# A gated scan and two feed-forward layers on one core: the first tile's blocks in a new order

## The chip, the cores and the metric

The kernel runs on 1 core of one Trainium2 chip. The metric is the device time of one execution in microseconds (us). Before the change the median of 3 runs is 1988.1 us (1988.08 to 1988.46).

## What is computed

```python
# x, f_logit: (2, 6080, 256) float32; lower_bound: (256,)
f = lower_bound + (1 - lower_bound) * sigmoid(f_logit)
h = 0
for t in range(6080):                 # one state per sequence and channel
    h = f[:, t] * h + (1 - f[:, t]) * x[:, t]
    y[:, t] = h
y = y.reshape(12160, 256)
h1 = y @ w_in1                        # 256 x 2048
y1 = (h1 - tanh(h1)) @ w_out1         # 2048 x 256
h2 = y1 @ w_in2
out = max(0.01 * h2, h2) @ w_out2
```

All of it is float32. Each float32 product is made of three matmuls: an operand is split into a rounded part (`_hi`) and the rest (`_lo`), and hi*hi, hi*lo and lo*hi are summed in PSUM.

## The kernel before, in words

Channels lie on the partitions (256 channels are two halves, k = 0 and 1), tokens on the free axis. A tile holds the same stretch of tokens of both sequences, b = 0 (A) and b = 1 (B): 448 of each in the first tile, 512 in the 11 others. Layer 1 runs over tiles 0 to 11 and writes `y1` to HBM, layer 2 over tiles 12 to 22 and the last. The 2048 hidden channels are 8 groups of 2 x 128, f = 0 and 1. A group of a tile so has four blocks (f, b) of 128 hidden channels by one sequence's tokens: C11 = (0, 0), C22 = (1, 1), C21 = (1, 0), C12 = (0, 1), numbered 0 to 3 in this order (lines 29 and 30).

From tile 1 on, the four blocks of a group come from seven products of sums of weights and of inputs (`slot`, line 362). The first tile does without them: `plain_block` (line 427) makes a block of two half-blocks, one for each k, of three matmuls each, so eight products for a group. Its four blocks have four PSUM banks: `p_ps`, `q_ps` and the two of `x_ps`. Then, for each block:
- ScalarE takes tanh of the bank into `full` (`plain_bend`, L594);
- VectorE subtracts it from the bank (`make_plain_g`, L914), after which the bank is free for the next group;
- ScalarE rounds `full` to `g_hi` (`round_g`, L619);
- VectorE writes the rest to `g_lo` (`split_g`, L878);
- TensorE multiplies with `w_out` and adds to the four banks of `y_ps` (`outputs`, L346 to L348): two outputs of three matmuls for each block.

Weights come from HBM as float32 and are split too: `plain_w_round` (L522, L523) and `plain_w_split` (L884, L886) for the plain part of `w_in`, `wo_round` (L538) and `wo_split` (L906) for `w_out`. GpSimd makes the sums of `w_in` that later tiles want (`sum_weights`, L1048 to L1053), rounded and split by `sum_w_round` (L527) and `sum_w_split` (L892). SyncE issues the loads, in a written order (lines 241 to 272): `load_wi(n)` waits, from n = 3 on, for `sum_w_split(n - 3)`, because there are three staging buffers; `load_wo(n)`, from n = 2 on, for `wo_split(n - 2)`.

Every engine runs a list in a fixed order, written by hand as slots, one for each group. In the first tile (`plain_slot`, lines 449, 634 and 918) TensorE does for group g: C11, then the outputs of C11 of group g - 1, then C22 and its outputs, C21, C12. Slot 0 has no outputs; TensorE begins with `WARM` matmuls on zeros and puts `FILL` more between the blocks of sequence A and those of B (L447).

Ahead of it stands the scan of the first tile, unit by unit (a unit is a k and a b; `FIRST_ORDER` takes both units of sequence A first): load of logits and x (`first_unit`, line 201), tanh (`first_squash`, L492), the gate's scale and shift (`first_forget_gate`, L501), (gate - 1) * x (`drive_term`, L768), the scan (L782), rounding and split of the result (L549, L828). The units of the next tile are interleaved with slots 1 to 4: `squash` (L509), `forget_gate` (L515), `drive_term` and `scan`, and behind them in slots 5 and 6 `keep_states` and the sums of inputs (L796, L803, L810) that tile 1 wants; `x_round` (L572) and `x_split` (L822) follow in slot 7.

The 8 weights W21 of the first tile are kept in the places of `x_hi` and `x_lo` that T3 and T1 take in tile 1 (`w21_place`), so their rounding must wait for the last blocks that read them.

```python
            def plain_slot(g):                     # TensorE, L449
...
                else:
                    for c in (C11, C22, C21, C12):
                        plain_block(g, c)
                        outputs(0, g - 1, c, 0, W_FIRST)
                        outputs(0, g - 1, c, 1, W_FIRST)
```

Of the kernel before, what the change touches and what calls it, by code (L numbers as in the profile page):

```python
# [8 lines left out]
WARM = 34  # L9
GROUPS = 8  # L10
# [24 lines left out]

FIRST_ORDER = (0, 2, 1, 3)
X12 = T4
FIRST_DONE = {C11: 1, C21: 2, C22: 3, C12: 4}
FILL = 12


def gated_scan_ffn_kernel(
# [41 lines left out]
    def plain_count(g, c):  # L84
        return FIRST_DONE[c] if g == 0 else 4 * g + c + 1

# [8 lines left out]
    with ExitStack() as ctx:  # L95
# [36 lines left out]
        bound_in = sem("bound_in")  # L132
        consts_ready = sem("consts_ready")
# [43 lines left out]

        block = ctx.enter_context(nc.Block())

        @block.sync  # L180
        def _(sp):
# [61 lines left out]
            load_wi(0)  # L243
            first_unit(2)
            first_unit(3)
            load_wi(1)
# [10 lines left out]
            load_wo(4)  # L257
            load_wi(5)
            load_unit(1, 3)
            load_wo(5)  # L260
            load_wi(6)
            load_unit(2, 0)
            load_wo(6)
            load_wi(7)
            load_unit(2, 1)
            load_wo(7)
# [66 lines left out]
        def _(pe):  # L333
# [16 lines left out]
            def outputs(s, g, c, k, W):  # L350
                q = 8 * s + g
                if k == 0:
                    pe.wait_ge(g_split, 4 * q + c + 1)
# [8 lines left out]
            def slot(s, g):  # L362
# [19 lines left out]
                if second and g == 0:  # L382
                    pe.wait_ge(full_ready, 4 * (GROUPS - 1) + C21 + 1)
                elif second and g == 1:
                    pe.wait_ge(full_ready, 4 * (GROUPS - 1) + C12 + 1)
# [23 lines left out]
                if not (second and g == 0):  # L409
                    pe.wait_ge(c12_ready, n)  # L410
# [13 lines left out]
            def plain_bank(c):  # L424
                return {C11: p_ps[:, :W_FIRST], C22: q_ps[:, :W_FIRST], C21: x_ps[:, 0, :W_FIRST], C12: x_ps[:, 1, :W_FIRST]}[c]

            def plain_block(g, c):
                f, b = BLOCK_OF[c]
                bank = plain_bank(c)
                if g >= 1:  # L430
                    pe.wait_ge(full_ready, 4 * (g - 1) + c + 1)
                if f == 0:
                    weights = [(wi_hi[:, g, W11, :], wi_lo[:, g, W11, :]), (wi_hi[:, g, W12, :], wi_lo[:, g, W12, :])]
                else:
                    weights = [(w21_place(x_hi, g), w21_place(x_lo, g)), (wi_hi[:, g, W22, :], wi_lo[:, g, W22, :])]
                inputs = (X11, X21) if b == 0 else (X12, X22)
                for k in range(2):
                    hi, lo = weights[k]
                    i = inputs[k]
                    nc.tensor.matmul(bank, hi, x_hi[:, i, :W_FIRST], start=k == 0, stop=False)  # L440
                    nc.tensor.matmul(bank, hi, x_lo[:, i, :W_FIRST], start=False, stop=False)
                    mm = nc.tensor.matmul(bank, lo, x_hi[:, i, :W_FIRST], start=False, stop=k == 1)
                mm.then_inc(plain_done, 1)
# [4 lines left out]

            def plain_slot(g):  # L449
                pe.wait_ge(plain_w_ready, g + 1)  # L450
                if g == 0:
                    pe.wait_ge(x_ready, 2)
                    plain_block(g, C11)
                    plain_block(g, C21)
                    warm(FILL)
                    pe.wait_ge(x_ready, 4)
                    plain_block(g, C22)
                    plain_block(g, C12)
                else:
                    for c in (C11, C22, C21, C12):  # L460
                        plain_block(g, c)
                        outputs(0, g - 1, c, 0, W_FIRST)
                        outputs(0, g - 1, c, 1, W_FIRST)
# [7 lines left out]

            for g in range(GROUPS):
# [15 lines left out]
        def _(act):  # L488
# [7 lines left out]
            def first_forget_gate(i):  # L496
                j = FIRST_ORDER[i]
                if i == 0:
# [52 lines left out]
            def x_round(s, i):  # L551
                W = width(s)
                act.wait_ge(sums_ready, sums_count(s) + 3)
                if isinstance(s, int) and s == 1:
                    act.wait_ge(plain_done, plain_count(GROUPS - 1, C12 if i in (T4, X22) else C21))
# [33 lines left out]
            def plain_bend(g, c):  # L589
                bank = {C11: p_ps[:, :W_FIRST], C22: q_ps[:, :W_FIRST], C21: x_ps[:, 0, :W_FIRST], C12: x_ps[:, 1, :W_FIRST]}[c]  # L590
                act.wait_ge(plain_done, max(plain_count(g, c), plain_count(g, C22)) if g == 0 and c == C21 else plain_count(g, c))
                if g >= 1:
                    wait_split(g - 1, c)
                nc.scalar.activation(full[:, c, :W_FIRST], bank, ACT.Tanh).then_inc(bent_ready, 1)  # L594
# [6 lines left out]
            def wait_split(n, c):  # L601
                act.wait_ge(g_split, 4 * n + c + 1)

            def begun(s, g, back):
                return not (isinstance(s, int) and 8 * s + g < back)

            def bend(s, g, c, W):
                q = 8 * s + g
                wait_block(q, c)
                if begun(s, g, 1):  # L610
                    wait_split(q - 1, c)
                nc.scalar.activation(full[:, c, :W], block_source(g % 2, c, W), ACT.Tanh).then_inc(bent_ready, 1)  # L612

            def round_g(s, g, c, W):
                q = 8 * s + g
                act.wait_ge(full_ready, 4 * q + c + 1)
                if begun(s, g, 2):
                    act.wait_ge(g_used, 4 * (q - 2) + c + 1)
# [15 lines left out]
            def plain_slot(g):  # L634
                if g >= 1:
# [471 lines left out]
```

## Time and profile before

| | |
|---|---|
| median of 3 runs | 1988.1 us |
| the profiled execution | 1988.08 us, its span 1986.3 us |
| TensorE (PE) busy | 1969.9 us, 99% of the span |
| weight loads of TensorE (PEld) | 1632.2 us, 82% |
| VectorE (DVE) | 1586.6 us, 80% |
| ScalarE (ACT) | 1247.8 us, 63% |
| GpSimd (POOL) | 39.6 us, 2% |
| HBM | 36 GB/s over the span |

The span runs from the first to the last instruction of the program; the time of the execution holds 1.8 us more. All places in time below are counted from the start of the span. PE is the matmul part of TensorE. Matmuls are pipelined: their recorded ends overlap the starts of the next ones, so their pace is read from start to start.

### The profile page before, as it was taken

How to read it: one execution, taken by the hardware profiler on the slowest of the kernel's cores; microseconds unless marked ns; L12 is line 12 of the kernel's file. 1: busy time of each engine (PE TensorE's matmuls, PEld its weight loads, DVE VectorE, ACT ScalarE, POOL GpSimd, SP SyncE). 2: the span in 40 equal slices, each digit the busy share in tenths (PEclk: the TensorE clock that was granted, in tenths of full speed). 3: DMA queues.
4: the chain of work that ended last, by engine and by line, in shares of the span. 5: the costliest groups of instructions: out<-in, count | busy, mean ns of one | idle time of the engine just before them, and what ended most of it. 6: DMA issues, size and time to landing. Idle time of an engine off the chain costs nothing.

```text
span 1986.3 us, 28715 instructions
## 1 busy us (share of the span) xinstructions
PE 1969.9 (99%) x8710; PEld 1632.2 (82%) x8710; DVE 1586.6 (80%) x2481; ACT 1247.8 (63%) x2205; POOL 39.6 (2%) x69
## 2 busy tenths in 40 slices
PE   8999999999999999999999999999999999999999
PEld 6888888888888888888888888888888888888887
DVE  6788888888888888888788777787777877878776
ACT  5577777777777777777665455554555545545454
POOL 1200000000000000000110000000000000000000
PEclk9999999999999999999999999999999999999999
DMA  3210110101101011011021010110101101011000
GB/s 122 64 51 22 54 43 21 53 32 42 42 21 63 23 41 42 21 69 40 21 75 40 6 43 1 42 42 0 42 0 42 42 0 42 0 42 42 0 21 21
DMA packets 38216, 71.14 MB, mean 36 GB/s; under 512 B 3360, under 2 KB 5920, under 8 KB 38176
## 3 DMA queue, kind: packets, MB, share of 16 engines
q1 hardware_dynamic: 38176, 70.66, 10.5%
q8 instruction: 18, 0.29, 0.1%
q14 instruction: 22, 0.18, 0.0%
HBM read 45.75 MB, written 24.90 MB: 36 GB/s over the span
## 4 chain that ended last, share of the span: by engine, by line
PE 96%; DVE 2%; ACT 1%; issue 0%; DMA 0%; SPq 0%; ACTq 0%; DVEq 0%
PE y_ps L346 17%; PE y_ps L347 17%; PE y_ps L348 17%; PE x_ps L336 8%; PE x_ps L337 8%; PE x_ps L338 8%; PE q_ps L336 4%; PE q_ps L337 4%; PE q_ps L338 4%; PE p_ps L336 2%; PE p_ps L337 2%; PE p_ps L338 2%; DVE g_lo L878 1%; DVE full L914 0%; DVE raw L782 0%
## 5 line engine op out<-in xcount | busy, mean ns | idle before, releaser
L619 ACT CAST g_hi<-full 128x512 fp32r<-128x512 f32 (+1 forms) x768 | 473.0, 616 | 265.3 <-DVE full L872 106.6
L878 DVE TENSOR_TENSOR g_lo<-full,g_hi 128x512 fp32r<-128x512 f32 (+1 forms) x768 | 508.1, 682 | 139.0 <-ACT g_hi L619 134.8
L346 PE MATMUL y_ps<-g_hi,wo_hi 128*128 128x512 f32 (+1 forms) x1536 | 597.2, 389 | 8.8 <-DVE wo_lo L906 8.8
L348 PE MATMUL y_ps<-g_hi,wo_lo 128*128 128x512 f32 (+1 forms) x1536 | 595.8, 388 | 0.0
L347 PE MATMUL y_ps<-g_lo,wo_hi 128*128 128x512 f32 (+1 forms) x1536 | 595.7, 388 | 0.0
L576 ACT COPY part<-x_ps 128x512 f32<-128x512 f32 (+1 forms) x552 | 319.5, 579 | 237.8 <-PE x_ps L338 232.8
L346 PEld LDWEIGHTS y_ps<-g_hi,wo_hi 128*128 128x128 f32 x1536 | 288.9, 188 | 70.5 <-issue 10.6
L348 PEld LDWEIGHTS y_ps<-g_hi,wo_lo 128*128 128x128 f32 x1536 | 289.0, 188 | 57.2
L347 PEld LDWEIGHTS y_ps<-g_lo,wo_hi 128*128 128x128 f32 x1536 | 289.1, 188 | 56.8
L336 PE MATMUL x_ps<-x_hi,wi_hi 128*128 128x512 f32 (+1 forms) x736 | 286.6, 389 | 0.0
L337 PE MATMUL x_ps<-x_lo,wi_hi 128*128 128x512 f32 (+1 forms) x736 | 285.7, 388 | 0.0
L338 PE MATMUL x_ps<-x_hi,wi_lo 128*128 128x512 f32 (+1 forms) x736 | 285.7, 388 | 0.0
L612 ACT ACTIVATE full<-part 128x512 f32<-128x512 f32 x264 | 167.3, 634 | 79.8 <-DVE part L835 68.5
L872 DVE SCALAR_TENSOR_TENSOR full<-part 128x512 f32<-128x512 f32 (+1 forms) x288 | 196.3, 682 | 1.7
L842 DVE TENSOR_TENSOR part<-q_ps,part 128x512 f32<-128x512 f32 (+1 forms) x184 | 126.3, 686 | 88.5 <-PE q_ps L338 85.3
L861 DVE TENSOR_TENSOR full<-part,full 128x512 f32<-128x512 f32 x264 | 181.4, 687 | 8.2 <-ACT full L612 5.1
L336 PEld LDWEIGHTS x_ps<-x_hi,wi_hi 128*128 128x128 f32 x736 | 138.1, 188 | 31.0 <-ACT part L576 2.7
L338 PEld LDWEIGHTS x_ps<-x_hi,wi_lo 128*128 128x128 f32 x736 | 138.1, 188 | 28.1
L337 PEld LDWEIGHTS x_ps<-x_lo,wi_hi 128*128 128x128 f32 x736 | 138.2, 188 | 26.9
L835 DVE TENSOR_TENSOR part<-p_ps,part 128x512 f32<-128x512 f32 (+1 forms) x184 | 126.2, 686 | 35.8 <-PE p_ps L338 35.7
L336 PE MATMUL q_ps<-x_hi,wi_hi 128*128 128x512 f32 (+1 forms) x368 | 143.1, 389 | 0.8 <-DVE part L842 0.7
L338 PE MATMUL q_ps<-x_hi,wi_lo 128*128 128x512 f32 (+1 forms) x368 | 142.8, 388 | 0.0
(95 smaller groups left out, 1790.8 us busy)
## 6 DMA issues: line engine op xcount, KB each, us to landing
gate<-f_logit SPq DMA_DIRECT2D x44, 256.0 KB, 2.7
drive<-x SPq DMA_DIRECT2D x44, 256.0 KB, 2.9
y<-y_out SPq DMA_DIRECT2D x22, 512.0 KB, 2.8
raw<-y SPq DMA_DIRECT2D x22, 512.0 KB, 4.4
out<-y_out SPq DMA_DIRECT2D x21, 512.0 KB, 2.8
wi_stage<-w_in SPq DMA_DIRECT2D x16, 256.0 KB, 3.3
wo_stage<-w_out SPq DMA_DIRECT2D x16, 256.0 KB, 2.8
y_out<-f_logit SPq DMA_DIRECT2D x4, 224.0 KB, 4.6
```

The lines of the kernel that those rows point to most:

```text
L336: nc.tensor.matmul(bank, hi, x_hi[:, i, :W], start=start, stop=False, skip_group_check=True)
L337: nc.tensor.matmul(bank, hi, x_lo[:, i, :W], start=False, stop=False, skip_group_check=True)
L338: return nc.tensor.matmul(bank, lo, x_hi[:, i, :W], start=False, stop=stop, skip_group_check=True)
L346: nc.tensor.matmul(bank, hi, g_hi[:, g % 2, c, :W], start=start, stop=False, skip_group_check=True)
L347: nc.tensor.matmul(bank, hi, g_lo[:, g % 2, c, :W], start=False, stop=False, skip_group_check=True)
L348: return nc.tensor.matmul(bank, lo, g_hi[:, g % 2, c, :W], start=False, stop=stop, skip_group_check=True)
L576: nc.scalar.copy(part[:, par, i, :W], x_ps[:, par, :W]).then_inc(chain_copied, 1)
L612: nc.scalar.activation(full[:, c, :W], block_source(g % 2, c, W), ACT.Tanh).then_inc(bent_ready, 1)
L619: nc.scalar.copy(g_hi[:, g % 2, c, :W], full[:, c, :W]).then_inc(g_hi_ready, 1)
L861: ins = nc.vector.tensor_tensor(full[:, c, :W], h, full[:, c, :W], ALU.subtract)
L872: ins = nc.vector.scalar_tensor_tensor(out=full[:, c, :W], in0=h, scalar=LEAK, in1=h, op0=ALU.mult, op1=ALU.max)
L878: nc.vector.tensor_tensor(g_lo[:, par, c, :W], full[:, c, :W], g_hi[:, par, c, :W].bitcast(F32), ALU.subtract).then_inc(g_split, 1)
```

## The change

The blocks of the first tile are put in a new order, and every engine's list with them:
- In the slots 1 to 6 TensorE makes C11 and C21 (sequence A) of group g + 1 and C22 and C12 (sequence B) of group g; each is followed by the outputs of C11 and C21 of group g, and of C22 and C12 of group g - 1. `FIRST_BLOCKS` and `FIRST_OUTPUTS` list both orders; `made` and `used` turn a block into the count at which it is done.
- The start is cut into half-blocks: those that read X11 alone come first, then those with X21, then C11 and C21 of group 1, then the blocks of B. So that C11 and C21 of groups 0 and 1 can be there at once, group 1 has two banks of `y_ps` and two places of `part` for them.
- `WARM` goes from 34 to 24 and the 12 `FILL` matmuls go.
- The gate of unit 0 is made by VectorE (`first_gate`), and the load of `bound` is issued by ScalarE instead of SyncE.
- SyncE's order: `load_wi(1)` ahead of units 2 and 3, each `load_wo(n + 1)` ahead of `load_wi(n + 1)`, one place earlier than before.
- On ScalarE and VectorE `wo_round` and `wo_split` come for group g + 1 in slot g, the weights of `w_in` for group g + 2, the drive of the next tile at the end of slots 1 to 4, its scans in slots 2 to 5.
- GpSimd's sums of group g wait for block C22 of group g - 1 (for g = 0: C21 of group 1) instead of C22 of group g.
- `x_round` of tile 1 waits for the new counts.

The diff, cut to its core:

```diff
-WARM = 34
+WARM = 24
-FIRST_DONE = {C11: 1, C21: 2, C22: 3, C12: 4}
-FILL = 12
+FIRST_BLOCKS = [(0, C11), (0, C21), (1, C11), (1, C21), (0, C22), (0, C12)]
+FIRST_OUTPUTS = [(0, C11), (0, C21)]
+for _g in range(1, GROUPS - 1):
+    FIRST_BLOCKS += [(_g + 1, C11), (_g, C22), (_g + 1, C21), (_g, C12)]
+    FIRST_OUTPUTS += [(_g, C11), (_g - 1, C22), (_g, C21), (_g - 1, C12)]
...
+    def made(q, c):
+        return FIRST_BLOCKS.index((q, c)) + 1 if isinstance(q, int) and q < GROUPS else 4 * q + c + 1
...
+        def plain_bank(g, c):
+            if g == 1 and c in (C11, C21):
+                return y_ps[:, (C11, C21).index(c), 1, :W_FIRST]
...
# SyncE
-                if i == 0:
-                    sp.dma_start(bound[:, :], lower_bound).then_inc(bound_in, 16)
             first_unit(0)
             first_unit(1)
             load_wi(0)
+            load_wi(1)
             first_unit(2)
             first_unit(3)
-            load_wi(1)
...
             load_wo(2)
+            load_wo(3)
             load_wi(3)
-            load_wo(3)
+            load_wo(4)
             load_wi(4)
...
# TensorE
+            def first_slots():
+                pe.wait_ge(plain_w_ready, 1)
+                pe.wait_ge(x_ready, 1)
+                plain_half(0, C11, 0)
+                plain_half(0, C21, 0)
+                pe.wait_ge(x_ready, 2)
+                plain_half(0, C11, 1)
+                plain_half(0, C21, 1)
+                pe.wait_ge(plain_w_ready, 2)
+                plain_block(1, C11)
+                plain_block(1, C21)
+                pe.wait_ge(x_ready, 3)
+                plain_half(0, C22, 0)
+                plain_half(0, C12, 0)
+                pe.wait_ge(x_ready, 4)
+                plain_half(0, C22, 1)
+                plain_half(0, C12, 1)
+                plain_outputs(0, C11)
+                plain_outputs(0, C21)
             def plain_slot(g):
+                if g + 1 < GROUPS:
+                    pe.wait_ge(plain_w_ready, g + 2)
+                    plain_block(g + 1, C11)
+                    plain_outputs(g, C11)
+                plain_block(g, C22)
+                plain_outputs(g - 1, C22)
+                if g + 1 < GROUPS:
+                    plain_block(g + 1, C21)
+                    plain_outputs(g, C21)
+                plain_block(g, C12)
+                plain_outputs(g - 1, C12)
# ScalarE
             def plain_slot(g):
+                if g + 1 < GROUPS:
+                    plain_bend(g + 1, C11)
+                plain_round_g(g - 1, C12)
+                sum_w_round(g - 1)
...
+                plain_bend(g, C22)
+                if g + 1 < GROUPS:
+                    plain_round_g(g + 1, C11)
+                    wo_round(g + 1)
+                    plain_bend(g + 1, C21)
...
+                plain_round_g(g, C22)
+                if g + 2 < GROUPS:
+                    plain_w_round(g + 2)
...
+                plain_bend(g, C12)
+                if g + 1 < GROUPS:
+                    plain_round_g(g + 1, C21)
...
                 if g in (1, 2, 3, 4):
                     squash(1, g - 1)
                     forget_gate(1, g - 1)
...
+            act.dma_start(bound[:, :], lower_bound).then_inc(bound_in, 16)
             first_squash(0)
-            first_forget_gate(0)
             first_squash(1)
             first_forget_gate(1)
             plain_w_round(0)
             first_x_round(X11, 0, 0)
+            plain_w_round(1)
+            first_x_round(X21, 2, 1)
             first_squash(2)
...
# VectorE
+            def first_gate():
...
+                nc.vector.tensor_scalar(
+                    y_out[:, b, k, :W_FIRST], y_out[:, b, k, :W_FIRST], gate_scale[:, k:k + 1], gate_shift[:, k:k + 1],
+                    ALU.mult, ALU.add,
+                ).then_inc(first_gate_ready, 1)
             def plain_slot(g):
+                if g + 1 < GROUPS:
+                    make_plain_g(g + 1, C11)
+                split_plain_g(g - 1, C12)
+                sum_w_split(g - 1)
+                if g in (2, 3, 4, 5):
+                    scan(1, g - 2)
...
+                make_plain_g(g, C22)
+                if g + 1 < GROUPS:
+                    split_plain_g(g + 1, C11)
+                    wo_split(g + 1)
+                    make_plain_g(g + 1, C21)
...
+                split_plain_g(g, C22)
...
+                if g + 2 < GROUPS:
+                    plain_w_split(g + 2)
...
+                make_plain_g(g, C12)
+                if g + 1 < GROUPS:
+                    split_plain_g(g + 1, C21)
+                if g in (1, 2, 3, 4):
+                    drive_term(1, g - 1)
...
+            first_gate()
             drive_term(0, 0)
             scan(0, 0)
...
             first_x_split(X11, 0, 0)
             plain_w_split(0)
             first_x_split(X21, 2, 1)
+            plain_w_split(1)
             drive_term(0, 2)
...
+            make_plain_g(0, C11)
             first_x_split(X22, 3, 3)
+            make_plain_g(0, C21)
+            wo_split(0)
+            split_plain_g(0, C11)
+            split_plain_g(0, C21)
...
# GpSimd
-                    pool.wait_ge(plain_done, plain_count(g, C22))
+                    pool.wait_ge(plain_done, made(1, C21) if g == 0 else made(g - 1, C22))
```

## Rows read from the trace of the kernel before

**Rows 1.** The page: a costly group of TensorE, and the issues of w_in

```profile
L346 PE MATMUL y_ps<-g_hi,wo_hi 128*128 128x512 f32 (+1 forms) x1536 | 597.2, 389 | 8.8 <-DVE wo_lo L906 8.8
...
wi_stage<-w_in SPq DMA_DIRECT2D x16, 256.0 KB, 3.3
```

**Rows 2.** Waits of 0 to 110 us: who for whom, sum, times, longest

```profile
DVE drive L768 <- ACT gate L515: 14.3, 4, 3.6
...
PE y_ps L346 <- DVE wo_lo L906: 8.8, 5, 2.0
...
PE p_ps L440 <- DVE wi_lo L886: 1.1, 2, 0.6
```

**Rows 3.** Busy time by stretch

```profile
core 0: us, PE busy (x) PEld busy (x) DVE busy (x) ACT busy (x) POOL busy (x), PEclk, DMA share, GB/s
6.70:11.00 4.30, 4.30 (x21) 1.96 (x20) 4.10 (x8) 3.81 (x8) 0.00 (x0) 1.00 0.98 367
34.00:37.30 3.30, 3.16 (x9) 2.84 (x10) 1.60 (x3) 2.10 (x6) 0.00 (x0) 0.50 0.23 79
60.74:73.49 12.75, 10.23 (x48) 8.85 (x49) 8.10 (x15) 7.02 (x15) 1.76 (x4) 1.00 0.27 84
83.76:93.68 9.92, 9.92 (x50) 9.01 (x48) 8.21 (x15) 5.33 (x12) 2.46 (x4) 1.00 0.09 28
103.60:1986.00 1882.40, 1877.51 (x8305) 1556.09 (x8304) 1515.23 (x2361) 1187.86 (x2087) 21.34 (x32) 1.00 0.10 33
```

**Rows 4.** Timeline of TensorE: start, duration, line, what; idle before and its releaser

```profile
1.32 10.13 PE L447 MATMUL y_ps<-zeros 128*128 128x512 bf16 x34 [1.32 <-POOL zeros L1068]
...
11.10 0.55 PE L440 MATMUL p_ps<-x_hi,wi_hi 128*128 128x448 f32 x1
...
13.72 2.76 PE L447 MATMUL y_ps<-zeros 128*128 128x512 bf16 x12
...
16.13 0.55 PE L440 MATMUL q_ps<-x_hi 128*128 128x448 f32 x1
...
21.38 0.44 PE L346 MATMUL y_ps<-g_hi,wo_hi 128*128 128x448 f32 x1 [1.26 <-DVE wo_lo L906]
...
34.14 0.71 PE L346 MATMUL y_ps<-g_hi,wo_hi 128*128 128x448 f32 x1 [1.98 <-DVE wo_lo L906]
...
60.74 0.44 PE L346 MATMUL y_ps<-g_hi,wo_hi 128*128 128x448 f32 x1 [1.78 <-DVE wo_lo L906]
...
73.49 0.44 PE L346 MATMUL y_ps<-g_hi,wo_hi 128*128 128x448 f32 x1 [1.97 <-DVE wo_lo L906]
...
103.60 0.39 PE L336 MATMUL x_ps<-x_hi,wi_hi 128*128 128x512 f32 x1
```

**Rows 5.** The same timeline: ends of two stretches without a wait

```profile
83.76 0.37 PE L440 MATMUL p_ps<-x_hi,wi_hi 128*128 128x448 f32 x1
...
85.83 0.37 PE L347 MATMUL y_ps<-g_lo,wo_hi 128*128 128x448 f32 x1
...
104.28 0.36 PE L346 MATMUL y_ps<-g_hi,wo_hi 128*128 128x448 f32 x1
...
106.10 0.39 PE L336 MATMUL x_ps<-x_hi,wi_hi 128*128 128x512 f32 x1
```

**Rows 6.** Timelines of VectorE and ScalarE in the start, one later row

```profile
5.48 0.62 DVE L768 SCALAR_TENSOR_TENSOR full<-y_out,full 128x448 f32<-128x448 f32 x1 [1.78 <-DMA full<-x]
6.14 1.09 DVE L782 TENSOR_TENSOR_SCAN raw<-y_out,full 128x448 f32<-128x448 f32 x1
...
9.07 0.62 DVE L828 TENSOR_TENSOR x_lo<-raw,x_hi 128x448 fp32r<-128x448 f32 x1
...
9.81 0.55 DVE L886 TENSOR_TENSOR wi_lo<-wi_stage,wi_hi 128x384 fp32r<-128x384 f32 x1
...
78.83 0.81 DVE L886 TENSOR_TENSOR wi_lo<-wi_stage,wi_hi 128x384 fp32r<-128x384 f32 x1
...
6.00 0.58 ACT L492 ACTIVATE y_out<-y_out 128x448 f32<-128x448 f32 x1 [1.27 <-DMA y_out<-f_logit]
...
7.86 0.30 ACT L522 CAST x_hi<-wi_stage 128x128 fp32r<-128x128 f32 x1 [0.49 <-DMA wi_stage<-w_in]
```

More of the change, by code:

```diff
@@ L176, in gated_scan_ffn_kernel, with plain_full @@
         last_stored = sem("last_stored")
+        def plain_bank(g, c):
+            if g == 1 and c in (C11, C21):
+                return y_ps[:, (C11, C21).index(c), 1, :W_FIRST]
+            return {C11: p_ps[:, :W_FIRST], C22: q_ps[:, :W_FIRST], C21: x_ps[:, 0, :W_FIRST], C12: x_ps[:, 1, :W_FIRST]}[c]
+        def plain_full(g, c):
+            if g == 1 and c in (C11, C21):
+                return part[:, 0, (C11, C21).index(c), :W_FIRST]
+            return full[:, c, :W_FIRST]
         block = ctx.enter_context(nc.Block())
@@ L408, in slot @@
                     pe.wait_ge(x_ready, x_count(s) + 5)
-                if not (second and g == 0):
+                if second and g == 0:
+                    pe.wait_ge(full_ready, made(GROUPS - 1, C22))
+                else:
                     pe.wait_ge(c12_ready, n)
@@ L445, in warm, with plain_outputs @@
+            def plain_block(g, c):
+                ago = made_ago(g, c)
+                if ago is not None:
+                    pe.wait_ge(full_ready, made(*ago))
+                plain_half(g, c, 0)
+                plain_half(g, c, 1)
+            def plain_outputs(g, c):
+                for k in range(2):
+                    if g == 0 and c == C22:
+                        pe.wait_ge(full_ready, made(1, (C11, C21)[k]))
+                    outputs(0, g, c, k, W_FIRST)
             def warm(count):
@@ L470, in _ @@
             warm(WARM)
-            for g in range(GROUPS):
+            first_slots()
+            for g in range(1, GROUPS):
                 plain_slot(g)
@@ L589, in plain_bend, with plain_round_g @@
             def plain_bend(g, c):
[L590 to L594, printed above, removed]
+                act.wait_ge(plain_done, made(g, c))
+                ago = made_ago(g, c)
+                if ago is not None:
+                    act.wait_ge(g_split, made(*ago))
+                nc.scalar.activation(plain_full(g, c), plain_bank(g, c), ACT.Tanh).then_inc(bent_ready, 1)
+            def plain_round_g(g, c):
+                act.wait_ge(full_ready, made(g, c))
+                if g >= 2:
+                    act.wait_ge(g_used, used(g - 2, c))
+                nc.scalar.copy(g_hi[:, g % 2, c, :W_FIRST], plain_full(g, c)).then_inc(g_hi_ready, 1)
             def block_source(par, c, W):
@@ L601, in wait_split @@
             def wait_split(n, c):
-                act.wait_ge(g_split, 4 * n + c + 1)
-            def begun(s, g, back):
-                return not (isinstance(s, int) and 8 * s + g < back)
+                act.wait_ge(g_split, made(n, c))
             def bend(s, g, c, W):
@@ L731, in _ @@
             first_forget_gate(3)
+            plain_bend(0, C11)
             first_x_round(X12, 1, 2)
+            plain_bend(0, C21)
+            wo_round(0)
+            plain_bend(1, C11)
             first_x_round(X22, 3, 3)
-            for g in range(GROUPS):
+            plain_round_g(0, C11)
+            plain_w_round(2)
+            plain_round_g(0, C21)
+            plain_bend(1, C21)
+            wo_round(1)
+            plain_bend(0, C22)
+            plain_round_g(1, C11)
+            plain_bend(0, C12)
+            plain_round_g(1, C21)
+            plain_round_g(0, C22)
+            for g in range(1, GROUPS):
                 plain_slot(g)
@@ L1022, in _ @@
             scan(0, 3)
+            make_plain_g(0, C11)
             first_x_split(X22, 3, 3)
+            make_plain_g(0, C21)
+            wo_split(0)
+            split_plain_g(0, C11)
+            split_plain_g(0, C21)
+            plain_w_split(2)
+            make_plain_g(1, C11)
+            make_plain_g(1, C21)
+            wo_split(1)
+            split_plain_g(1, C11)
+            make_plain_g(0, C22)
+            split_plain_g(1, C21)
+            make_plain_g(0, C12)
+            split_plain_g(0, C22)
             keep_states(0)
-            for g in range(GROUPS):
+            for g in range(1, GROUPS):
                 plain_slot(g)
```

181 lines of the change are left out of this document (80 added, 101 removed).

## The prediction

> **What bounds the kernel now.** I read the page first: the costliest group of TensorE was idle for 8.8 us in the whole run, ended by `wo_split` [rows 1]. The waits of the first 110 us hold the same 8.8 us in 5 waits and 1.1 us in 2 waits for `plain_w_split` [rows 2]. So everything to be had lies in the first tile. Behind it, some 8305 matmuls take 1882.4 us, 0.2267 each, TensorE busy for 1877.5 of them [rows 3], and the change leaves their order alone. Any gain is made before tile 1 and carried unchanged to the end.
>
> The first tile runs from 11.10 to 103.60, where the first three-part product of tile 1 starts [rows 4]: 92.5 us. It has 64 half-blocks and 56 outputs of three matmuls each, 360 in all (24 more outputs run inside tile 1, before and after the change). Their pace, start to start, is 2.07 us for ten in one stretch and 1.82 for nine, 0.202, in another [rows 5]; I take 0.2045 each, so 73.6 us of work. 18.9 us are lost. Where:
> - 12 filling matmuls on zeros, 13.72 to 16.13: 2.4 us [rows 4].
> - Five waits of the outputs: idle 8.8 us; a stall also costs the 0.16 us by which a matmul's end lies behind its successor's normal start (0.36 less 0.20 [rows 5]), so 9.6. Two waits for weights: 1.1 + 2 x 0.16 = 1.4 [rows 2, 4].
> - Three stretches with a granted clock of 0.50, the 1.2 GHz level instead of 2.4. One stands in [rows 3]: 9 matmuls in 3.3 us, 0.37 each, so 9 x 0.168 = 1.5 us lost; the other two look alike, 4.6 together. Each follows one of the long waits, which end at 34.14, 47.43 and 73.49 [rows 4].
> - The rest, 0.9, is slow first matmuls behind stalls.
>
> Why TensorE waits is seen in the slot from 60.74 to 73.49: 12.75 us long, yet VectorE is busy only 8.10 and ScalarE 7.02. The slot from 83.76 to 93.68 has VectorE at 8.21, ScalarE at 5.33, and 9.92 us for the same 48 matmuls without a stall [rows 3]. Neither engine is full; the order makes them wait on each other. In slots 1 to 4 VectorE's `drive_term` stands in line for ScalarE's gate (14.3 us in 4 waits [rows 2]), and behind it everything up to `wo_split`, for which the outputs wait.
>
> **The start, part by part.** The bound's load leaves SyncE's queue, so the x load of unit 0, issued at 1.67, goes 0.48 earlier; first_gate moves that gate from ScalarE to VectorE. VectorE waited for x, not for the gate, until 5.48 [rows 6], so moving the gate is worth nothing: both engines idle there. The earlier issue is worth between 0 and 0.45 us. I take 0.2. The two loads run side by side on the same transfers as before. The Trainium skill ("DMA: Bandwidth & Descriptors", section "Issuing engines are not separate DMA queues") says that starting DMAs from several engines saves only the sequencer's time to initiate. By that rule the worth would be this 0.48 us of issue at most; no row of before shows a second issuer.
>
> From there I walk the two queues, each instruction behind its queue and its wait, with the durations of [rows 6] (drive and splits 0.62, scan 1.09; in a full queue the next starts 0.08 before a record ends). Drive 5.3, scan 5.9 to 7.0; ScalarE squash 6.0, gate 6.6 to 7.4 (it waits for the logits, landed at 6.00 [rows 6]); drive 7.4, scan 8.1 to 9.15. ScalarE rounds the weights of group 0 at 7.9 (landed then [rows 6]) and X11 at 8.5. VectorE splits X11 at 9.1 and the weights until 10.4. TensorE then starts with 6 half-blocks' matmuls on X11 alone, 0.15 to 0.2 behind that, at 10.5; 10.3 with the earlier landing. Before, it stood behind X21 too: 11.10. The 24 warming matmuls hand over near 9.0 (before, 34 did at 11.1, and ten at the fillers' 0.21 go [rows 4]), so a gap of 1.3 us opens here. It is no work and costs nothing, if the clock holds.
>
> VectorE goes on without a gap: X21 split by 10.9, weights 1 by 11.6 (their load goes out right behind group 0's now; units 2 and 3 come 256 KB later, some 0.7 us at the 370 GB/s of [rows 3], and are needed only at 10.1 and later), drive and scan of unit 2 to 13.25, X12 split by 14.5, scan 3 to 15.5, make C11, X22 split by 16.7, make C21, `wo_split(0)`, split C11 by 18.4. TensorE has 30 matmuls ahead of X22: 10.5 + 6.1 = 16.6, waits 0.2; six more, 18.1; waits 0.4 for split C11; 12 outputs, 21.1. The wait of [rows 4] for the first outputs and the filler are gone. Stalls here: 0.6 plus 0.2 for slow firsts.
>
> **The slots.** A slot keeps its 48 matmuls, 9.8 us, and the other engines keep their work (8.1 and 7.0 us in the worst kind of slot [rows 3]); it is only ordered otherwise. C11 and C21 of group g+1 are computed a slot ahead of their outputs, `wo_split` no longer stands behind `make` of C21, the drive stands last in the slot and its scan in the next. Walking both queues on, slot 1's outputs find their splits done 0.3 to 0.8 us ahead, later ones 2 us and more, the weights about 1 us. The tightest place is group 3's weights. `sum_w_split(0)` ends near 25.8, SyncE issues the load, 3.1 to 3.3 us until landing [rows 1], round 0.7 and split 0.75: 30.5, against slot 2's start at 30.9. Late by the whole spread, it would cost 0.5. SyncE's queue: `load_wo(3)` now stands ahead of `load_wi(3)`, but its condition `wo_split(1)` is met near 21; so for later pairs. GpSimd's sums move a block or more earlier (for g = 0 behind C21 of group 1, near 15), still beside VectorE: there a weight split took 0.81 instead of 0.55 [rows 6]. One or two such in a slot with 1.7 us to spare are hidden, save in the start and at group 3, for which I put 0.3 us. The x rounds of tile 1 now wait for other blocks; X11 is split near 82.6 and wanted at 85: covered.
>
> **The sum.** 10.3 + 73.6 + 0.8 + 0.3 = 85.0, against 103.6: 18.6 us earlier. As a cross-check: losses of 2.4 + 9.6 + 1.4 + 4.6 + 0.9 gone, 0.8 at the start, and 1.1 comes back. The profiled execution took 1988.08 (span 1986.3 and 1.8 around it), the median of the runs is 1988.1. So 1988.1 - 18.6 = **1969.5 us**. A measurement here tells about 0.2%, 4.0 us.
>
> **Rivals.**
> - **Half clock at the start.** The falls of the clock followed idles of 1.98 and 1.97 us (and the one that ends at 47.43, close to them); none followed 1.26 or 1.78 [rows 4]; the new gap of 1.3 between warming and X11 is 1.0 as these rows count idle. If the clock falls there, 9 matmuls lose 1.5 us: 1971.0. Chance 0.12. The Trainium skill ("TensorE: Matmul & The Clock Gate", Part 1) says that the warm-up is a matter of time and not of a number of matmuls, and that the moment varies between runs. By that rule cutting the warming to 24 is safe only where the clock has risen by 9.0; in this trace 34 took 10.1 us where 0.21 each is the fast pace [rows 4], so some 13 ran at 0.43, up to about 6.8; the trace agrees, with room for 2 us.
> - **The two helpers become the bound.** If their instructions ran 0.1 us longer each in the new order (beside GpSimd 0.26 longer for one kind [rows 6]), the start has 20 in a row (+2) and the weights come late in slots 2 to 6 (+2): near 89, so 1973.5. Against it: the slot of 9.92 us with VectorE 8.21 busy beside GpSimd. Chance 0.15.
> - **The order doesn't do what it says.** The four long waits return behind another instruction, clock falls with them: only the filler (2.4), the start (0.8) and the first wait (1.4) are won: 1983.5. For it: the queues stay strictly in order on both engines. Against: walked in the same way, the old order gives its own waits within 0.2 us each. Chance 0.06.
> - **Slower: the pace of the matmuls.** It is 2% slower from 83.76 than in tile 1 from 104.28, for matmuls of the same 448 columns [rows 5], and no row shows why. If the new start locked the tiles behind it into the slower pace, 1882 us become 1920: +38 - 18.6, so 2007.5. It decides from half of the tiles on (18.6/38). Against it: the pace came back by itself once tile 1 ran, and the tiles' own order is untouched. Chance 0.02.
>
> **How the numbers follow.** The forecast has 0.65; its own range goes from 1968.4 (x another 0.25 earlier, pace 0.203, nothing late for 0.3) to 1971.0 (no earlier landing, 0.5 for the weights, pace 0.2067), and a little beyond on either side for what a walk leaves out. The range given, 1967.0 to 1974.5, takes in the first two rivals. Faster: 0.65 + 0.12 + 0.15 and half of the third rival, whose 4.6 us are at the bound, 0.95; within 0.2%: 0.03; slower: 0.02.
>
> **What would show it.** First real matmul near 10.4, on half-blocks; no wait on `wo_split` of 1 us or more; a clock that never falls between 6.7 and the end; `product` of tile 1 first at 85; 8304 matmuls in 1882 us behind it. Wrong: waits of TensorE in slots 1 to 6 that sum to more than 2 us, a half clock stretch inside the tile, or a tile 1 that takes back part of it.

## The result, and the profile after

The changed kernel takes 1970.35 us in the median of 4 runs (1969.44 to 1971.84) against 1988.09; the ratio is 0.9912, 95% interval [0.9894, 0.9929]. Five more runs of it later gave 0.9913 [0.9900, 0.9927], median 1970.77. The forecast was 1969.5 with a range of 1967.0 to 1974.5.

The profiled execution took 1969.44 us, its span is 1967.6. First the page, then the waits of TensorE up to 95 us and stretches of it; they answer to [rows 1], [rows 2] and [rows 3]. The outputs' line L346 is L372 now, the blocks' lines L440 to L442 are L462 to L464.

```profile
span 1967.6 us, 28678 instructions
PE 1959.2 (100%) x8688; PEld 1626.8 (83%) x8688; DVE 1587.0 (81%) x2482; ACT 1247.4 (63%) x2204; POOL 47.5 (2%) x69
L372 PE MATMUL y_ps<-g_hi,wo_hi 128*128 128x512 f32 (+1 forms) x1536 | 595.7, 388 | 0.7 <-DVE g_lo L1015 0.7
```

```profile
PE p_ps L462 <- DVE wi_lo L982: 0.9, 1, 0.9
PE y_ps L372 <- DVE g_lo L1015: 0.7, 1, 0.7
PE q_ps L462 <- DVE x_lo L924: 0.3, 1, 0.3
```

```profile
core 0: us, PE busy (x) PEld busy (x) DVE busy (x) ACT busy (x) POOL busy (x), PEclk, DMA share, GB/s
10.50:21.00 10.50, 9.50 (x44) 8.15 (x45) 10.23 (x17) 8.20 (x17) 5.00 (x8) 1.00 0.48 177
30.90:40.60 9.70, 9.70 (x50) 8.99 (x49) 8.76 (x15) 6.96 (x15) 3.33 (x4) 1.00 0.34 108
40.60:50.40 9.80, 9.80 (x50) 9.09 (x49) 8.48 (x14) 7.06 (x15) 3.33 (x4) 1.00 0.33 108
85.36:1967.60 1882.24, 1877.08 (x8305) 1556.37 (x8303) 1513.68 (x2359) 1188.00 (x2086) 21.33 (x32) 1.00 0.10 33
```

Read the first number behind the bar of L372: 8.8 us of idle time have become 0.7, and `wo_split` is no releaser any more. The two full slots take 9.7 and 9.8 us for their 48 matmuls where [rows 3] had 12.75, with VectorE (8.76 and 8.48 us) and ScalarE (6.96 and 7.06) as busy as before or a little busier: nothing became lighter, it is only ordered. The clock column is 1.00 in every stretch. Behind the first tile the same matmuls take 1882.2 us to the end of the span, against 1882.7 before (1986.3 less 103.60; the stretch of [rows 3] stops at 1986.00).

TensorE's timeline shows where the first tile begins, waits and ends (for [rows 4]), and VectorE's shows why it still waits:

```profile
7.70 1.89 PE L483 MATMUL y_ps<-zeros 128*128 128x512 bf16 x8
10.47 0.47 PE L462 MATMUL p_ps<-x_hi,wi_hi 128*128 128x448 f32 x1 [0.88 <-DVE wi_lo L982]
...
17.11 0.47 PE L462 MATMUL q_ps<-x_hi,wi_hi 128*128 128x448 f32 x1 [0.29 <-DVE x_lo L924]
...
19.32 0.47 PE L372 MATMUL y_ps<-g_hi,wo_hi 128*128 128x448 f32 x1 [0.71 <-DVE g_lo L1015]
...
85.36 0.39 PE L362 MATMUL x_ps<-x_hi,wi_hi 128*128 128x512 f32 x1
```

```profile
4.74 0.63 DVE L864 SCALAR_TENSOR_TENSOR full<-y_out,full 128x448 f32<-128x448 f32 x1
...
7.24 0.63 DVE L864 SCALAR_TENSOR_TENSOR full<-y_out,full 128x448 f32<-128x448 f32 x1 [0.75 <-ACT y_out L554]
...
16.17 0.88 DVE L924 TENSOR_TENSOR x_lo<-raw,x_hi 128x448 fp32r<-128x448 f32 x1
16.98 0.61 DVE L1009 TENSOR_TENSOR full<-x_ps,full 128x448 f32<-128x448 f32 x1
17.51 0.95 DVE L1002 TENSOR_TENSOR wo_lo<-wo_stage,wo_hi 128x512 fp32r<-128x512 f32 x1
18.38 1.68 DVE L1015 TENSOR_TENSOR g_lo<-full,g_hi 128x448 fp32r<-128x448 f32 x2
```

Tile 1 starts at 85.36 instead of 103.60, 18.24 us earlier; the rest of the 18.6 us between the two profiled executions lies in the 1882 us behind it. From here on the place of tile 1's first product is the measure, because medians of a few runs carry a spread of a microsecond. It is the place in one execution, though, and the same kernel came out at 85.36 and at 86.38, so a difference counts only together with the waits that explain it. Waits are given as the idle time in brackets in the rows. Counted from start to start they are 0.16 us longer each, because a matmul's recorded end lies behind the normal start of the next.

### The profile page after: what moved, and what is told of

It is laid out like the page before. It is cut to its first block, busy times and chain, and to the rows that moved or that the text cites. A ratio compares the mean times of both kernels' runs of the same rounds, so it can differ in the third digit from the quotient of the medians.

```text
span 1967.6 us, 28678 instructions
## 1 busy us (share of the span) xinstructions
PE 1959.2 (100%) x8688; PEld 1626.8 (83%) x8688; DVE 1587.0 (81%) x2482; ACT 1247.4 (63%) x2204; POOL 47.5 (2%) x69
## 4 chain that ended last, share of the span: by engine, by line
PE 98%; DVE 1%; ACT 0%; DMA 0%; SPq 0%; issue 0%; DVEq 0%
PE y_ps L372 18%; PE y_ps L373 17%; PE y_ps L374 17%; PE x_ps L362 8%; PE x_ps L363 8%; PE x_ps L364 8%; PE q_ps L362 4%; PE q_ps L363 4%; PE q_ps L364 4%; PE p_ps L364 2%; PE p_ps L363 2%; PE p_ps L362 2%; DMA wi_stage<-w_in 0%; PE x_ps L463 0%; PE x_ps L462 0%; PE x_ps L464 0%
## 5 line engine op out<-in xcount | busy, mean ns | idle before, releaser
L680 ACT CAST g_hi<-full 128x512 fp32r<-128x512 f32 (+1 forms) x736 | 454.8, 619 | 226.0 <-DVE full L968 106.7
L974 DVE TENSOR_TENSOR g_lo<-full,g_hi 128x512 fp32r<-128x512 f32 (+1 forms) x736 | 487.6, 683 | 135.5 <-ACT g_hi L680 131.4
L372 PE MATMUL y_ps<-g_hi,wo_hi 128*128 128x512 f32 (+1 forms) x1536 | 595.7, 388 | 0.7 <-DVE g_lo L1015 0.7
L372 PEld LDWEIGHTS y_ps<-g_hi,wo_hi 128*128 128x128 f32 x1536 | 288.3, 188 | 61.1 <-DVE g_lo L974 2.7
```

Of the source, the lines that this page charges most:

```text
L372: nc.tensor.matmul(bank, hi, g_hi[:, g % 2, c, :W], start=start, stop=False, skip_group_check=True)
L680: nc.scalar.copy(g_hi[:, g % 2, c, :W], full[:, c, :W]).then_inc(g_hi_ready, 1)
L974: nc.vector.tensor_tensor(g_lo[:, par, c, :W], full[:, c, :W], g_hi[:, par, c, :W].bitcast(F32), ALU.subtract).then_inc(g_split, 1)
```

## The experiments

**Why TensorE waited: the place of the drive, and sequence A a group ahead.** Each of the two alone. First the kernel before with only ScalarE's and VectorE's work for the next tile moved:

```diff
 # ScalarE, plain_slot of the kernel before
                 if g + 1 < GROUPS:
                     plain_w_round(g + 1)
-                if g in (1, 2, 3, 4):
-                    squash(1, g - 1)
-                    forget_gate(1, g - 1)
...
+                if g in (1, 2, 3, 4):        # last in the slot
+                    squash(1, g - 1)
+                    forget_gate(1, g - 1)
 # VectorE
-                    if g in (1, 2, 3, 4):
-                        drive_term(1, g - 1)
                     split_g(g - 1, 1 - par, C12, W_FIRST)
                     sum_w_split(g - 1)
+                    if g in (2, 3, 4, 5):
+                        scan(1, g - 2)
...
+                if g in (1, 2, 3, 4):        # last in the slot
+                    drive_term(1, g - 1)
```

> The kernel before with one part of the change alone: on ScalarE squash and forget_gate of the next tile stand at the end of slots 1 to 4, on VectorE drive_term stands at the end of the slot and the scan in the next slot; TensorE's order, the start, the warming and the loads stay as before. Theory (VectorE's drive_term waiting for the gate holds up everything behind it): the two queues walked with this order give waits of 1.4, 0.2, 1.4, 1.4 and 2.6 us for wo_split and none for the weights, and the first product of tile 1 at 95.7, plus 0 to 3 us for falls of the clock: time 1980 to 1984, about 40% of the gain. Rival (only computing sequence A a group ahead removes the waits): still four waits near 2 us, 103 and 1987 to 1988. Second rival (this part is the whole gain): 88 and 1972.

1983.3 us in the median, ratio 0.9975 [0.9965, 0.9985], tile 1 at 98.08. The waits of VectorE and TensorE up to 105 us:

```profile
DVE drive L768 <- ACT gate L515: 3.1, 4, 0.8
...
PE y_ps L346 <- DVE wo_lo L906: 7.4, 5, 2.5
PE p_ps L440 <- DVE wi_lo L886: 0.3, 1, 0.3
```

Its longest wait is the only one with half clock behind it, from 78.1 to 81.5:

```profile
78.02 0.63 PE L346 MATMUL y_ps<-g_hi,wo_hi 128*128 128x448 f32 x1 [2.47 <-DVE wo_lo L906]
```

The wait for the gate fell from 14.3 to 3.1 us [rows 2], yet the outputs still waited for `wo_split`: 7.4 us, where it had been 8.8. The theory's place came out (95.7 plus up to 3), and so did its waits: 1.31, 0.30, 1.67, 1.68 and 2.47 us of idle time, where it had 1.4, 0.2, 1.4, 1.4 and 2.6; one small wait for the weights it had not named. The places that the two rivals gave, 103 and 88, are both out. What the first rival says is right in part, though: most of the waiting for `wo_split` stays without the new order of the blocks. This part is 5.5 of the 18.2 us, 30% where about 40% was expected, and only 2.2 of the 5.5 are shorter waits (7.7 us for 9.9). The clock fell once here and three times in the kernel before; at 1.5 us a fall, the two that are gone are some 3.1 us, an estimate from the stretches at half clock.

Then the new kernel with that part undone. It keeps everything else of the change, the start and the loads too, and not the order of the blocks alone:

```diff
 # ScalarE
                 plain_bend(g, C22)
+                if g in (1, 2, 3, 4):
+                    squash(1, g - 1)
+                    forget_gate(1, g - 1)
...
 # VectorE
                     make_plain_g(g + 1, C11)
+                if g in (1, 2, 3, 4):
+                    drive_term(1, g - 1)
                 split_plain_g(g - 1, C12)
                 sum_w_split(g - 1)
-                if g in (2, 3, 4, 5):
-                    scan(1, g - 2)
...
                 make_plain_g(g, C22)
+                if g in (1, 2, 3, 4):
+                    scan(1, g - 1)
```

> The new kernel with one part undone: squash and forget_gate of the next tile stand inside slots 1 to 4 again (behind plain_bend of C22), VectorE's drive_term stands ahead of the split of C12 and the scan in the same slot. TensorE's order with sequence A a group ahead, the start and the loads stay new. Theory (the order of the blocks and the place of the drive are both needed): the outputs never wait, but the weights of the next group come late, four waits of TensorE of 2.7 us for plain_w_split, in slots 2 to 5, first product of tile 1 at 95.8 plus up to 6 us of fallen clock: 1980 to 1986. Rival (with A a group ahead the place of the drive no longer matters): below 87 and 1971.

1985.2 us, ratio 0.9988 [0.9979, 0.9998], tile 1 at 101.20. Waits of VectorE and TensorE up to 105 us, and two rows of SyncE's and ScalarE's timelines:

```profile
DVE drive L864 <- ACT gate L568: 12.8, 4, 3.8
...
PE p_ps L462 <- DVE wi_lo L982: 10.1, 5, 2.5
...
PE y_ps L372 <- DVE g_lo L1015: 0.5, 1, 0.5
```

```profile
29.80 0.33 SPq L216 DMA_DIRECT2D wi_stage<-w_in  x1
...
32.52 0.30 ACT L575 CAST x_hi<-wi_stage 128x128 fp32r<-128x128 f32 x1 [1.61 <-DMA wi_stage<-w_in]
```

No wait for `wo_split` is left, as the new order of the blocks promises, but the drive, waiting for its gate for 12.8 us again, holds `sum_w_split` behind it, which releases the staging buffer for the next load, and the load is issued at 29.80 where the new kernel has it at 27.1. It is used at 32.52, 2.7 us behind its issue, and TensorE waits for it, slot after slot: 2.25, 2.44, 2.37 and 2.52 us, where 2.7 were expected, with a stretch at half clock at each of the first three. So the place of the drive alone wins 5.5 us (98.08), everything else alone 2.4 us (101.20), and the two together 18.2. Both patterns of waits came out as the walk of the queues had them, each wait that was named within 0.5 us. Not named were a wait of 0.82 us for X22, 0.29 in the new kernel, and one of 0.47 for the first outputs.

**What the filler cost.** The kernel before without it:

```diff
                     plain_block(g, C21)
-                    warm(FILL)
                     pe.wait_ge(x_ready, 4)
```

> The kernel before without its 12 filling matmuls. The prediction booked them as 2.4 us of lost time. Theory now: they hid a wait for the split of X22, which ended at 16.07, and the next block began at 16.13, so without them TensorE just stands idle for 2.4 us: first product of tile 1 at 103.6, time 1988, or 1.5 more (1989.6) if this idle makes the clock fall once. As the prediction had it: 101.2 and 1985.7.

Nothing, by the time: 1988.48 us, ratio 1.0002 [0.9993, 1.0011]. Its timeline of TensorE has an idle in the filler's place, up to the same block at almost the same time as in [rows 4] (16.13 there):

```profile
13.28 0.37 PE L442 MATMUL x_ps<-x_hi,wi_lo 128*128 128x448 f32 x1
16.02 0.47 PE L440 MATMUL q_ps<-x_hi 128*128 128x448 f32 x1 [2.37 <-DVE x_lo L827]
...
59.51 0.71 PE L346 MATMUL y_ps<-g_hi,wo_hi 128*128 128x448 f32 x1 [1.98 <-DVE wo_lo L905]
...
102.52 0.47 PE L336 MATMUL x_ps<-x_hi,wi_hi 128*128 128x512 f32 x1 [0.86 <-DVE x_lo L821]
```

The 2.4 us were a wait for X22 with matmuls on zeros laid over it. In the new kernel X22 is split even later (17.05 against 16.07), and the gain lies in the real matmuls that stand ahead of it, 30 where the old order had 12. Tile 1 came at 102.52 in this execution, between the two places of the expectation. That isn't the filler's worth: the clock fell only once here, near 59.5, where it fell three times in the kernel before (some 3.1 us), and the waits behind 20 us were 1.6 us longer in sum. The median of ten executions is within 0.4 us of the kernel before's.

**The loads.** Two edits of the new kernel's start:

```diff
 # wi1_back
             load_wi(0)
-            load_wi(1)
             first_unit(2)
             first_unit(3)
+            load_wi(1)
 # bound_back: the load of bound on SyncE again, behind unit 0's logits
+                if i == 0:
+                    sp.dma_start(bound[:, :], lower_bound).then_inc(bound_in, 16)
...
-            act.dma_start(bound[:, :], lower_bound).then_inc(bound_in, 16)
```

> The new kernel with load_wi(1) behind units 2 and 3 again, nothing else. Group 1's weights land near 11.3 instead of 8.9, and ScalarE's plain_w_round(1) stands ahead of the round of X21 in its queue. Theory (walk of the queues): TensorE's second half-blocks wait 1.4 us for X21, the later waits are 0.9 for X22 and 0.4 for the first outputs; first product of tile 1 2.3 us later than in the new kernel, time 1972.6. Rival (weights 1 are not needed so early): within 0.5 us of the new kernel.

> The new kernel with the load of bound on SyncE's queue again, ahead of the x load of unit 0. In the new kernel that x landed at 4.04 instead of 5.35, but the next thing VectorE needs, the gate of unit 1, is ready at 7.24 only. Theory (this part is worth nothing): x lands near 5.4, drive at 5.4, scan until 7.15, the drive of unit 1 at 7.24 to 7.4 as before, first real matmul within 0.15 us of 10.5. Rival: it moves by 0.45 us or more.

`wi1_back`: tile 1 at 87.26, 1.9 us later, 1971.6 us. The mechanism is as expected: ScalarE stands for the weights and X21 behind them, and TensorE waits 1.20 us for X21, 1.08 for X22 and 0.17 and 0.30 for outputs, where the new kernel waited 0.29 and 0.71:

```profile
11.15 0.30 ACT L575 CAST x_hi<-wi_stage 128x128 fp32r<-128x128 f32 x1 [2.19 <-DMA wi_stage<-w_in]
```

`bound_back`: the first real matmul at 10.55 against 10.47, so the part is worth nothing to it, because VectorE waits for the gate of unit 1 either way. VectorE's two drives there:

```profile
5.12 0.63 DVE L865 SCALAR_TENSOR_TENSOR full<-y_out,full 128x448 f32<-128x448 f32 x1 [0.65 <-DMA full<-x]
...
7.12 0.62 DVE L865 SCALAR_TENSOR_TENSOR full<-y_out,full 128x448 f32<-128x448 f32 x1 [0.25 <-ACT y_out L556]
```

Its one execution showed something else, though. Stretches of it:

```profile
4.20:7.80 3.60, 3.60 (x18) 1.57 (x16) 2.63 (x5) 1.34 (x2) 0.00 (x0) 1.00 0.94 277
7.80:10.50 2.70, 0.25 (x2) 0.00 (x0) 2.37 (x5) 2.51 (x7) 0.00 (x0) 1.00 1.02 370
11.00:14.30 3.30, 3.30 (x11) 2.89 (x10) 2.84 (x6) 2.12 (x4) 0.00 (x0) 0.50 1.06 398
```

The warming matmuls start 0.43 us apart at first and 0.21 us apart later; where that changes, the clock has risen (the clock column reads 1.00 ahead of it too). Here it rose at 4.2 already (it did at 6.7 and 7.3 in the profiles of before and after), so the 24 warming matmuls were over at 8.05. TensorE stood until 10.55, 2.50 us, and the clock fell to the 1.2 GHz level for 3.4 us. Tile 1 came at 86.37, 1.0 us later than in the profile after, at the same pace of the matmuls behind the fall. This is the prediction's first rival.

**The warming, halved and lengthened.** `WARM` 12 and 31 instead of 24, and the new kernel again:

```diff
-WARM = 24
+WARM = 12        # warm12; warm31: WARM = 31
```

> The new kernel once more, for its spread. Four runs of it gave 1969.4, 1971.0, 1971.8 and 1969.7, with a mean granted clock of 1.000 in the two short ones and 0.999 in the two long ones; the kernel before stood at 0.997 each time, which is its three stretches at half clock. Theory (the clock falls once in some executions, in the gap of about 1.1 us between warming and the first real matmul or in the waits behind it): again two groups of times, some 1.5 to 2.4 us apart, the longer ones with 0.999. Rival (the spread has nothing to do with the clock): times spread without the clock differing.

> WARM 31 instead of 24, nothing else, so the gap ahead of the first real matmul is closed (24 warming matmuls end at 9.3 by the pace, seven more at 0.2135 end at 10.8; the first real one was ready at 10.5). Theory (the gap is what lets the clock fall in some executions): the first real matmul about 0.3 us later, the first product of tile 1 at 85.4 to 85.7, all times within 1 us of each other near 1969.7 and every mean clock at 1.000. Rival (the falls come from the two waits at 17 and 19 us, or from the chip): the spread stays, 1969.5 to 1972, with 0.999 in some.

> The new kernel with WARM 12 instead of 24. The profile of the variant with bound on SyncE's queue showed one fall: the clock rose at 4.14, so the 24 warming matmuls were through at 7.9, TensorE stood until 10.55, and the clock was at half from 10.97 to 14.38. Theory (the gap between warming and the first real matmul is what makes the clock fall): with 12 the gap is 3.5 to 4 us in every execution, so the first real matmuls run at half clock every time; nine of them at 0.37 lose 1.5 us, of which the wait for X22 gives back 0.5: first product of tile 1 near 86.4 to 87, times 1971 to 1972.5, none below 1970.5. Rival (the gap doesn't matter): as the new kernel, 1969.4 to 1972 with some executions below 1970.

`warm12`: 1971.56 us, 1970.95 to 1972.01, a mean granted clock of 0.998 in all five executions, tile 1 at 87.69. Its stretches:

```profile
7.50:10.70 3.20, 0.00 (x0) 0.00 (x0) 2.59 (x5) 3.07 (x8) 0.00 (x0) 0.86 1.03 367
10.70:14.00 3.30, 2.94 (x8) 2.63 (x9) 3.27 (x7) 2.19 (x4) 0.00 (x0) 0.50 1.05 398
14.00:17.40 3.40, 3.40 (x13) 3.04 (x12) 1.94 (x4) 2.05 (x4) 0.00 (x0) 0.61 0.14 52
```

Behind the gap of 4.5 us the clock fell, here for 6.8 us; the other four executions have the same mean clock, so it seems to have fallen in each. The 15 matmuls at 0.37 lose 2.5 us and the start is 0.6 later; the place moves by 2.3, so the waits for X22 and the first outputs take up the rest. The place is 0.7 us beyond what was expected, the times are inside. `new_again`: 1970.45 to 1971.99. `warm31`: 1969.45 to 1971.11, median 1970.15. So the spread stayed with the gap closed, and its expectation of 1 us failed. In the two profiled executions of the new kernel, 1969.44 and 1970.60 us, it is no fall of the clock, of which neither has one before its last microseconds, but the matmuls' own pace, which moved tile 1 from 85.36 to 86.38. For the executions without a profile that isn't shown. Ten steps in the middle of the same slot, in the profile after and in `new_again`:

```profile
50.10 0.36 PE L372 MATMUL y_ps<-g_hi,wo_hi 128*128 128x448 f32 x1
...
52.12 0.36 PE L463 MATMUL p_ps<-x_lo,wi_hi 128*128 128x448 f32 x1
```

```profile
50.42 0.37 PE L372 MATMUL y_ps<-g_hi,wo_hi 128*128 128x448 f32 x1
...
52.48 0.37 PE L463 MATMUL p_ps<-x_lo,wi_hi 128*128 128x448 f32 x1
```

**GpSimd beside VectorE.** The sums of groups 0 and 1 later:

```diff
-                    pool.wait_ge(plain_done, made(1, C21) if g == 0 else made(g - 1, C22))
+                    if g == 0:
+                        pool.wait_ge(g_used, 1)
+                    elif g == 1:
+                        pool.wait_ge(plain_done, made(2, C11))
+                    else:
+                        pool.wait_ge(plain_done, made(g - 1, C22))
```

> The new kernel with GpSimd's sums of groups 0 and 1 later: group 0 waits for the first outputs (g_used 1, near 20.5) instead of block C21 of group 1 (15.7), group 1 for block C11 of group 2 (near 23) instead of C22 of group 0 (18.1). Nothing else. Theory (GpSimd slows VectorE where VectorE is the bound: between 16.2 and 20.5 a split took 0.88 and 0.84 instead of 0.62, wo_split 0.95 instead of 0.68, a small weight split 0.54 instead of 0.28, 1.4 us in all): the waits ahead of X22 and of the first outputs shrink from 0.45 and 0.87 to 0.25 and 0.45, so the first product of tile 1 comes 0.6 us earlier, or less where the load of group 3's weights is late then. In time 1969.8 against 1970.4, at the edge of what five rounds tell; the VectorE durations tell it. Rival (the longer durations have another cause): VectorE's durations between 16 and 20 stay.

VectorE's timeline of it, the same instructions as in the profile after:

```profile
16.55 0.62 DVE L924 TENSOR_TENSOR x_lo<-raw,x_hi 128x448 fp32r<-128x448 f32 x1
17.10 0.62 DVE L1009 TENSOR_TENSOR full<-x_ps,full 128x448 f32<-128x448 f32 x1
17.63 0.68 DVE L1002 TENSOR_TENSOR wo_lo<-wo_stage,wo_hi 128x512 fp32r<-128x512 f32 x1
18.23 1.15 DVE L1015 TENSOR_TENSOR g_lo<-full,g_hi 128x448 fp32r<-128x448 f32 x2
```

0.88, 0.95 and 1.68 have become 0.62, 0.68 and 1.15, so the lengthening is GpSimd's; the instruction that reads PSUM, L1009, took 0.61 beside it too. The wait for the first outputs fell from 0.71 to 0.18 us (0.88 to 0.35 from start to start). The place did not move by the 0.6 us expected, it is 85.36 again: this execution began at 10.56, 0.1 later, and a new wait of 0.17 us (0.34 from start to start) for group 3's weights ended at 31.75. GpSimd's sums now run in slot 1, and the split of sums ahead of the load of those weights took 0.95 us there for 0.68. 1970.0 us, ratio 0.9913 [0.9900, 0.9927], is the new kernel's time.

Both parts that looked better in a trace together:

```diff
-WARM = 24
+WARM = 31
 # and the edit of pool_late
```

> The two parts that looked better in a trace together: GpSimd's sums of groups 0 and 1 later, and WARM 31. Theory: no fall of the clock (1.000 in all), the wait for the first outputs near 0.35 instead of 0.87, a wait of 0.3 for group 3's weights; first product of tile 1 at 85.2 with the fast pace and 86.3 with the slow one, times 1969.3 to 1970.6. Rival (what is left of the spread is the matmuls' pace alone, and the two parts cancel): indistinguishable from the new kernel's 1969.4 to 1972.

1969.54 us (1968.77 to 1970.22, 4 runs), ratio 0.9909 [0.9894, 0.9924], tile 1 at 85.18, where 85.2 was expected. It is the lowest median of all, 0.8 us under the new kernel's, and its interval overlaps the new kernel's: if it is better, then by too little to be told here.

## Why the prediction was right, point by point

- **Place and kind of the gain.** Everything in the first tile, carried unchanged to the end: 18.24 of 18.6 us lie before tile 1's first product. 85.0 was forecast for it, the profile has 85.36, its repetition 86.38. That the first is so near is in part luck: the start came 0.2 us later than forecast and the stalls were 0.8 too small, and a fast pace, which another execution didn't have, gave 0.6 back.
- **The long waits and the falls behind them** (9.6 + 1.4 + 4.6 us): gone, as forecast. The reason given for the waits of before, that the drive's wait for the gate holds up everything behind it, was only a part of it. `before_drives` takes that away and keeps 7.7 of 9.9 us of waits; `drives_back` keeps the drive's wait and waits for the weights instead of `wo_split`. The prediction's walk had the new order of the blocks as well, and both are needed.
- **The filler, 2.4 us**, was booked as a cost of its own. It was none (`before_nofill`): the term was a wait for X22 and belonged with the stalls. The sum was not hurt, since the new order puts real matmuls in the same place.
- **The start.** 10.3 was forecast, 10.47 measured. The 0.2 us for the earlier x landing was not earned: the next gate and the weights' landing were later than it. The x came earlier by more than its earlier issue, as the drive ran at 4.74 without a wait, where before it waited until 5.48 [rows 6]. So the bound that the prediction took from the Trainium skill ("DMA: Bandwidth & Descriptors", "Issuing engines are not separate DMA queues"), 0.48 us of issue, was too low for how much earlier the x came, and too high for what that was worth, which is nothing.
- **Stalls of the start and slots, 1.1 us forecast**: 1.9 measured, the one term that was clearly too small. 10.47 + 360 x 0.2027 = 83.4, and 85.36 is 1.9 behind it. VectorE's instructions beside GpSimd were longer by 0.26, 0.27 and twice 0.26, of which 0.3 had been set aside. It is the second rival in small: it cost 0.5 us at the first outputs (0.88 from start to start against 0.35 in `pool_late`) where 4 were feared: no later slot of the profile has a wait of TensorE.
- **Pace.** 0.2045 was assumed between two observed levels. The profile had 0.2027 for the whole tile (0.6 us less than forecast), the repetition 0.2067 from 19.6 on (0.7 us more).
- **Half clock at the start**, chance 0.12, priced at 1.5 us: it exists, `bound_back` shows it at 1.0 us, and `warm12` shows it behind a longer gap. The prediction ordered the falls by the length of the idle ahead, and that doesn't hold: `before_nofill` idled for 2.37 us at 16.02 without a fall. The Trainium skill's rule ("TensorE: Matmul & The Clock Gate", Part 1) that the moment of the rise varies between executions is borne out: it was at 4.2 (`bound_back`), 5.8 (`late_and_31`), 6.7 (before) and 7.3 us (after). The same rule says that it is a matter of time and not of a number of matmuls, and that no run here can tell, since all of them warm with the same matmuls. How many of the nine executions of the new kernel had a fall stays open: a mean clock of 0.999 was found in six of them, but also in the profiled execution of `late_and_31`, where no fall lies before the last microseconds.
- **Slower through the pace of the tiles**: did not happen; 1882.2 to 1882.8 us from tile 1 to the end of the span in every profile of the new kernel and its variants.

## What to carry to other kernels

When a trace shows engines that wait on each other and none is full, walk the queues with the trace's own durations: it told the waits that it named in four orders to within half a microsecond each, and that two edits were needed together. How often the clock would fall it did not tell, and that was worth up to 4.6 us here. Look at what a filler covers before booking it as a cost, and put into its place work that doesn't need the late operand. In the start of a kernel, price each VectorE instruction that runs beside GpSimd by its longer form, and keep the warming matmuls until the first real ones are ready.

## What the runs showed of the hardware that I had not expected

- Matmuls of 448 columns run at one of two steady paces at the same granted clock of 1.00, 0.2027 or 0.2067 us from start to start, and keep it for tens of microseconds. In these traces the pace changed at waits, where the clock came back, or where the width of the matmuls changed: 0.2027 to 0.2067 behind the wait that ended at 19.1 in `new_again`, at 23.5 in `warm31`, and back in tile 1 in both; in the kernel before the slow pace set in behind the last stretch at half clock (78.4). It is worth 1.3 us in a first tile, as much as the parts tried above, and the same kernel had it either way. What sets it stays open.
- The clock fell around short idles, and the length of the idle alone didn't tell whether it would. It fell around idles of 1.84, 1.97 and 1.98 us in the kernel before, 2.47 in `before_drives`, 2.25, 2.37 and 2.44 in `drives_back`, 1.98 in `before_nofill`, 2.50 in `bound_back` and 4.48 in `warm12`. It did not fall around 1.78 us in the kernel before, around 1.78, 1.95, 1.98 and 2.37 in `before_nofill`, and around 2.52 in `drives_back`. What the engine did ahead of each differs too, so these are cases and no rule.
- The load of bound, 1 KB, ahead of the x load of 224 KB on one queue made VectorE wait for x until 5.12 (`bound_back`) and 5.48 [rows 6]; without it the drive ran at 4.74, right behind its gate (ready at 4.71), without a wait for x, and the x load was issued only 0.48 us earlier.
